# Layer two of a fused kernel: from four blocks of 384 tokens to three of 512, with three pieces of block zero one position later

## The reference, cut to what matters

```
recurrence:  y = mLSTM(q, k, v, input gate, forget gate, output gate)      # per head, over 768 steps
layer one:   x1 = (sigmoid(y @ wg) * (y @ wv)) @ wo                        # 320 -> 1536 -> 320
layer two:   xn = x1 / sqrt(mean(x1 * x1) + 1e-6) * g
             out = (a * sigmoid(a) * (xn @ wv2)) @ wo2    with a = xn @ wg2
```

## Time and profile before

| | |
|---|---|
| median of three runs | 476.69 us (476.38 to 476.94) |
| the profiled execution's own time | 475.81 us |
| its span, first to last instruction | 474.1 us |
| granted TensorE clock, mean | 0.996 |
| layer one's first hidden matmul | 22.66 us |
| layer two's first matmul | 280.88 us |
| layer two's last matmul begins | 471.02 us |

### The profile page before, as it was taken

How to read it: one execution, slowest core, us unless ns; L and a number is a source line. 1 busy time by engine, 2 the same in 40 slices (tenths; PEclk the granted TensorE clock), 3 DMA queues, 4 the chain that set the end, 5 groups by cost and what they waited for, 6 DMA issues and landing times.

```text
span 474.1 us, 9969 instructions
## 1 busy us (share of the span) xinstructions
PE 467.4 (99%) x4115; PEld 455.1 (96%) x4115; DVE 236.0 (50%) x515; ACT 201.0 (42%) x407; POOL 104.1 (22%) x144
## 2 busy tenths in 40 slices
PE   8999999999999999999999999999999999999997
PEld 3899989999999999999999999999999999999997
DVE  8848865562866175435534525650455045504550
ACT  7878446623462636154416743430243024302430
POOL 5979910211101110100014967000000000000000
PEclk9899999999999999999999999999999999999999
DMA  7674720211122012101141520000000100010001
GB/s 245 211 244 145 177 64 29 63 44 43 44 74 61 1 45 58 46 1 35 67 151 52 182 85 1 2 15 29 1 1 7 37 1 3 4 39 2 1 4 39
DMA packets 11475, 27.92 MB, mean 59 GB/s; under 512 B 1526, under 2 KB 5830, under 8 KB 11430
## 3 DMA queue, kind: packets, MB, share of 16 engines
q1 hardware_dynamic: 11110, 27.20, 18.3%
q10 hardware_dynamic: 320, 0.08, 0.1%
HBM read 25.23 MB, written 1.97 MB: 57 GB/s over the span
## 4 chain that ended last, share of the span: by engine, by line
PE 89%; POOL 5%; DVE 3%; ACT 1%; DMA 1%; issue 1%; POOLq 0%; ACTq 0%
PE bank L1055 27%; PE bank L1006 10%; PE bank L1007 9%; PE bank L1075 9%; PE bank L1077 8%; PE bank L1076 8%; PE bank L1009 6%; PE bank L954 3%; PE bank L927 2%; POOL wgv_lo L415 2%; PE bank L1085 2%; PE bank L874 2%; PE bank L946 1%; POOL wgv_hi L418 1%; DMA raw_x<-in_w_o 1%; PE bank L905 1%
## 5 line engine op out<-in xcount | busy, mean ns | idle before, releaser
L1006 PE MATMUL bank<-x_hi,wgv_hi 128*128 128x256 f32 x432 | 121.1, 290 | 0.3 <-DVE x_lo L786 0.3
L1007 PE MATMUL bank<-x_lo,wgv_hi 128*128 128x256 f32 x432 | 118.0, 283 | 0.0
L609 ACT ACTIVATE sg<-bank 128x256 f32<-128x256 f32 (+1 forms) x120 | 51.1, 426 | 151.8 <-PE bank L1007 74.9
L1075 PE MATMUL bank<-wo_hi,h_hi 128*128 128x320 f32 x288 | 90.1, 313 | 0.0
L829 DVE TENSOR_TENSOR hf<-sg,bank 128x256 f32<-128x256 f32 (+1 forms) x120 | 56.7, 473 | 65.1 <-ACT sg L609 62.1
L1055 PE MATMUL bank<-x_hi,wgv_hi 64*128 64x384 f32 x576 | 89.0, 333 | 0.0
L1077 PE MATMUL bank<-wo_hi,h_lo 128*128 128x320 f32 x288 | 89.0, 309 | 0.0
L1076 PE MATMUL bank<-wo_lo,h_hi 128*128 128x320 f32 x288 | 89.0, 309 | 0.0
L1006 PEld LDWEIGHTS bank<-x_hi,wgv_hi 128*128 128x128 f32 x432 | 82.7, 191 | 1.5 <-DVE x_lo L786 0.4
L1007 PEld LDWEIGHTS bank<-x_lo,wgv_hi 128*128 128x128 f32 x432 | 82.7, 191 | 0.0
L1009 PE MATMUL bank<-x_hi,wgv_lo 128*128 128x256 f32 x288 | 81.5, 283 | 0.0
(11 more groups left out here) (125 smaller groups left out, 516.9 us busy)
## 6 DMA issues: line engine op xcount, KB each, us to landing
step<-in_w_gv SPq DMA_DIRECT2D x7, 576.0 KB, 3.8
step<-in_vok SPq DMA_DIRECT2D x12, 324.0 KB, 3.6
step<-in_qk_t SPq DMA_DIRECT2D x24, 160.0 KB
raw_x<-in_w_gv SPq DMA_DIRECT2D x5, 576.0 KB, 4.9
raw_p<-in_w_gv SPq DMA_DIRECT2D x4, 576.0 KB, 4.8
y<-y_tok SPq DMA_DIRECT2D x12, 160.0 KB, 1.8
step<-in_vok SPq DMA_DIRECT2D x10, 180.0 KB, 4.5
step<-in_q_t SPq DMA_DIRECT2D x10, 180.0 KB, 2.5
```

Source lines behind the costliest of these rows:

```text
L609: act.activation(sg[:, f % 2, 0:w], g_view(lay, n), ACT.Sigmoid).then_inc(sg_done, 1)
L1006: pe.matmul(ps, wgv_hi[:, wc, s, cs], x_hi[:, xs, s, :], start=(s == 0), stop=False)
L1007: mm = pe.matmul(ps, wgv_hi[:, wc, s, cs], x_lo[:, xs, s, :], start=False, stop=(s == 2))
L1075: pe.matmul(ps, h[0][:, f, ts], wo_hi[:, f, :], start=(f == 0), stop=False)
```

## The change

Layer two takes four tiles, 512 tokens, per block, in three blocks. The inner values of 512 tokens need more room: f = 0 to 8 stay in `h_hi` and `h_lo`, f = 9 to 11 go to `d_rhs` (high) and to the place of the second `step` buffer (low), and `hf` of layer two goes to the place of `d_lhs`. The fourth projected tile goes out through `num`. As the second `step` buffer is written early in layer two, the weight chunks use the buffers in another order (`RAW1`): chunks 8 and 11 use `raw_p`, so chunk 11 is loaded when chunk 8 is split (before: when chunk 6 was). The last two O pieces stand behind the first and second projected tile of block zero, in banks 0 and 1, and a second or third block waits for both at its start. In block zero of layer one, T of tile 3 moves from slot 12 to slot 13 (on DVE between sub-steps 2 and 3 of A), F of position 2 from slot 13 to 14 and R from slot 14 to 15. The diff, cut:

```diff
-T1 = 3
+T1 = 4
 N1 = T1 * P
 NB1 = NT // T1
+HF = 9
...
 FIRST = [[], [("S", 2)], [], [("K", 2), ("N", 2)], [("Y", 2)], [("D", 3)], [], [("S", 3), ("T", 2)], [],
-         [("K", 3), ("N", 3)], [("Y", 3)], [], [("T", 3), ("A", 2, 0), ("A", 2, 1)],
-         [("A", 2, 2), ("A", 2, 3), ("A", 2, 4), ("F", 2)], [("R", 2)], []]
+         [("K", 3), ("N", 3)], [("Y", 3)], [], [("A", 2, 0), ("A", 2, 1)],
+         [("A", 2, 2), ("T", 3), ("A", 2, 3), ("A", 2, 4)], [("F", 2)], [("R", 2)]]
...
-        h_hi = sb("h_hi", [P, NF * N1], F32R)
-        h_lo = sb("h_lo", [P, NF * N1], F32R)
+        h_hi = sb("h_hi", [P, HF * N1], F32R)
+        h_lo = sb("h_lo", [P, HF * N1], F32R)
...
-        hf = sb("hf", [P, 2, N1], F32)
-        y_tok = sb("y_tok", [P, T1, 3 * P], F32)
+        hf = sb("hf", [P, 2 * N0], F32)
+        y_tok = sb("y_tok", [P, 1 + B, 3 * P], F32)
...
+            over("pad_step", [P, QK + QT + VOK], F32)
+            more_lo = over("more_lo", [P, QK + QT + VOK], F32R)
+            over("pad_rhs", [P, R, P], F32R)
+            hf1 = over("hf1", [P, 2 * N1], F32)
         step = [sb(f"step{b}", [P, QK + QT + VOK], F32) for b in range(B)]
         d_rhs = sb("d_rhs", [P, R, P], F32R)
...
+        more = [d_rhs[:, :, :].rearrange("p r t -> p (r t)"), more_lo]
+        RAW1 = [0, 1, 2, 3, 4, 0, 1, 2, 4, 0, 1, 4]
+
+        def h_view(lay, low, f):
+            t = (h_hi, h_lo)[low]
+            if lay == 0:
+                return t[:, f * N0:(f + 1) * N0]
+            return t[:, f * N1:(f + 1) * N1] if f < HF else more[low][:, (f - HF) * N1:(f - HF + 1) * N1]
...
+        def y_out(t):
+            return y_tok[:, t, 0:DM] if t <= B else num[:, 0:DM]
...
+        def o_bank(n):
+
+            return bank[7] if n < NT - B else bank[n - (NT - B)]
...
             def load_raw1(c):
-                s = c % len(raw1)
-                if c >= len(raw1):
-                    sp.wait_ge(split1, c - len(raw1) + 1)
+                s = RAW1[c]
+                if s in RAW1[0:c]:
+                    sp.wait_ge(split1, c - RAW1[0:c][::-1].index(s))
...
                 for t in range(T1):
-                    if k == 0 and t < B:
-                        piece(("O", NT - B + t))
                     act.wait_ge(o_done, NT + T1 * k + t + 1)
...
-                    act.activation(y_tok[:, t, 0:DM], o_view(1, T1 * k + t), ACT.Copy).then_inc(oe_done, 1)
+                    act.activation(y_out(t), o_view(1, T1 * k + t), ACT.Copy).then_inc(oe_done, 1)
+                    if k == 0 and t < B:
+                        piece(("O", NT - B + t))
...
-                    if n == NT - B:
-
-                        pe.wait_ge(hf_done, F1 + NF - 2)
-                    turn(bank[7], 1 + n % B).then_inc(ot_done, 1)
+                    if n >= NT - B:
+
+                        pe.wait_ge(hf_done, F1 + NF - 1)
+                    turn(o_bank(n), 1 + n % B).then_inc(ot_done, 1)
...
-                            pe.wait_ge(x2_done, max(T1 * (k + 1), NT - B))
+                            pe.wait_ge(x2_done, NT if k else NT - B)
...
                         else:
-                            pe.wait_ge(x2_done, NT)
                             pe.wait_ge(oe_done, T1 * k)
...
                 for t in range(T1):
-                    if k == 0 and t < B:
-
-                        piece(("O", NT - B + t))
                     for half in range(2):
                         project(1, k, t, half)
+                    if k == 0 and t < B:
+                        piece(("O", NT - B + t))
```

More of the change, by code:

```diff
@@ L112, in mlstm_moe_kernel @@
                 first.append(under(f"first{b}", [P, NF * N0], F32R))
-                tails.append(under(f"tail{b}", [P, NF * (N1 - N0)]))
+                tails.append(under(f"tail{b}", [P, HF * N1 - NF * N0]))
         x_hi = sb("x_hi", [P, NT, 3, P], F32R)
         x_lo = sb("x_lo", [P, NT, 3, P], F32R)
-        h_hi = sb("h_hi", [P, NF * N1], F32R)
-        h_lo = sb("h_lo", [P, NF * N1], F32R)
+        h_hi = sb("h_hi", [P, HF * N1], F32R)
+        h_lo = sb("h_lo", [P, HF * N1], F32R)
         wgv_hi = sb("wgv_hi", [P, GVC, 3, CW], F32R)
@@ L122, in mlstm_moe_kernel @@
         raw_p = sb("raw_p", [P, 3 * CW], F32)
-        sg = sb("sg", [P, 2, N1], F32)
-        hf = sb("hf", [P, 2, N1], F32)
-        y_tok = sb("y_tok", [P, T1, 3 * P], F32)
+        sg = sb("sg", [P, 2 * N1], F32)
+        hf = sb("hf", [P, 2 * N0], F32)
+        y_tok = sb("y_tok", [P, 1 + B, 3 * P], F32)
         g_row = sb("g_row", [P, DM], F32)
@@ L130, in mlstm_moe_kernel, with over @@
         QK, QT, VOK = 2 * NG * P + 2 * P, NG * P, HE + DM + KN
+        with ExitStack() as late:
+            def over(name, shape, dt):
+                return late.enter_context(nc.sbuf_tensor(name, shape, dt))
+            over("pad_step", [P, QK + QT + VOK], F32)
+            more_lo = over("more_lo", [P, QK + QT + VOK], F32R)
+            over("pad_rhs", [P, R, P], F32R)
+            hf1 = over("hf1", [P, 2 * N1], F32)
         step = [sb(f"step{b}", [P, QK + QT + VOK], F32) for b in range(B)]
@@ L167, in mlstm_moe_kernel, with sg_view, hf_view @@
         raw1 = [step[s // 2][:, s % 2 * 3 * CW:(s % 2 + 1) * 3 * CW] for s in range(4)] + [raw_p[:, :]]
-        h0 = [t[:, 0:NF * N0].rearrange("p (f t) -> p f t", t=N0) for t in (h_hi, h_lo)]
-        h1 = [t[:, :].rearrange("p (f t) -> p f t", t=N1) for t in (h_hi, h_lo)]
+        more = [d_rhs[:, :, :].rearrange("p r t -> p (r t)"), more_lo]
[5 more added lines that the diff above has]
+            return t[:, f * N1:(f + 1) * N1] if f < HF else more[low][:, (f - HF) * N1:(f - HF + 1) * N1]
+        def sg_view(lay, f):
+            w = (N0, N1)[lay]
+            return sg[:, f % 2 * w:(f % 2 + 1) * w]
+        def hf_view(lay, f):
+            w = (N0, N1)[lay]
+            return (hf, hf1)[lay][:, f % 2 * w:(f % 2 + 1) * w]
+        def y_out(t):
+            return y_tok[:, t, 0:DM] if t <= B else num[:, 0:DM]
         bank = [ctx.enter_context(nc.psum_tensor(f"bank{i}", [P, 512], F32)) for i in range(8)]
@@ L190, in raw_of @@
         def raw_of(lay, c):
-            ring = (raw0, raw1)[lay]
-            r = ring[c % len(ring)]
+            r = raw0[c % len(raw0)] if lay == 0 else raw1[RAW1[c]]
             if c < GVC:
@@ L376, in _ @@
                     row = m % B * S + m // B * P
-                    sp.dma_start(out[row:row + P, :], y_tok[:, t, 0:DM]).then_inc(out_sent[t], 16)
+                    sp.dma_start(out[row:row + P, :], y_out(t)).then_inc(out_sent[t], 16)
             for t in range(T1):
@@ L513, in high @@
             def high(lay, c):
-                ring, whi = ((raw0_in, whi0), (raw1_in, whi1))[lay]
-                s = c % len(ring)
-                act.wait_ge(ring[s], 16 * (c // len(ring) + 1))
+                whi = (whi0, whi1)[lay]
+                if lay == 0:
+                    act.wait_ge(raw0_in[c % len(raw0)], 16 * (c // len(raw0) + 1))
+                else:
+                    act.wait_ge(raw1_in[RAW1[c]], 16 * RAW1[0:c + 1].count(RAW1[c]))
                 if c < GVC:
@@ L571, in piece @@
                     act.wait_ge(ot_done, n + 1)
-                    act.activation(x_hi[:, n, :, :], t_view(bank[7]), ACT.Copy).then_inc(xh2_done, 1)
+                    act.activation(x_hi[:, n, :, :], t_view(o_bank(n)), ACT.Copy).then_inc(xh2_done, 1)
             act.wait_ge(consts, 1)
@@ L604, in sigmoid @@
             def sigmoid(lay, n, f):
-                w = (N0, N1)[lay]
                 act.wait_ge(g_done if lay else v_done, n + 1)
@@ L608, in sigmoid @@
                     act.wait_ge(hf_done, n - 1)
-                act.activation(sg[:, f % 2, 0:w], g_view(lay, n), ACT.Sigmoid).then_inc(sg_done, 1)
+                act.activation(sg_view(lay, f), g_view(lay, n), ACT.Sigmoid).then_inc(sg_done, 1)
             def h_high(lay, n, f):
-                w, h = ((N0, h0), (N1, h1))[lay]
                 act.wait_ge(hf_done, n + 1)
@@ L618, in h_high @@
                         act.wait_ge(o_done, before)
-                act.activation(h[0][:, f, :], hf[:, f % 2, 0:w], ACT.Copy).then_inc(hhi_done, 1)
+                act.activation(h_view(lay, 0, f), hf_view(lay, f), ACT.Copy).then_inc(hhi_done, 1)
             for k in range(NB0):
@@ L650, in _ @@
                 for t in range(T1):
-                    if k == 0 and t < B:
-                        piece(("O", NT - B + t))
                     act.wait_ge(o_done, NT + T1 * k + t + 1)
-                    if k == 0 and t:
+                    if k == 0 and 0 < t <= B:
                         act.wait_ge(ot_done, NT - B + t)
@@ L789, in piece @@
                     dve.wait_ge(xh2_done, n + 1)
-                    dve.tensor_tensor(x_lo[:, n, :, :], t_view(bank[7]), x_hi[:, n, :, :].bitcast(F32),
+                    dve.tensor_tensor(x_lo[:, n, :, :], t_view(o_bank(n)), x_hi[:, n, :, :].bitcast(F32),
                                       ALU.subtract).then_inc(x2_done, 1)
@@ L819, in gate @@
             def gate(lay, n, f):
```

(20 more changed lines are left out.)

## The result

| | median, us | runs |
|---|---|---|
| before | 476.79 | 476.38 to 476.94 (4) |
| after | 472.63 | 472.42 to 474.14 (4) |
| ratio | 0.9921 | 95% interval 0.9899 to 0.9942 |

The kernel is 4.2 us faster; 4.9 were forecast (471.8), and the time lies in the range. The interval of the ratio allows 2.8 to 4.8.

The account below looks back on a forecast made before the run. PE, busy for 99% of the span, was taken to bound the kernel. Gains of 2.9 + 2.0 = 4.9 us took 475.81 to 470.9, or 471.8 us with the median's 0.9 carried over; range 470.5 to 474.3.

Parts of the forecast that it names:

- The step of 512 columns: Layer two's pairs: a step takes 213.3 + 14.5 = 227.8 ns, the excess belonging to the instruction.
- Rival (a): Layer two's pairs: the excess grows with the columns, 232.7 ns a step, time 474.5 us; chance 0.10.
- (c): Layer two's pairs: halves writing two whole banks cost more, slower than before from 238.6 ns a step; chance 0.04.
- part one: Layer two at 512 columns: 540 steps instead of 720, gain 2.9 us, 2.7 of it in the steps.
- Layer two: All of layer two: three blocks plus the two O pieces take 187.6 us, against 190.47 before.
- ACT and DVE beside it: Longer tiles in layer two: multiply 689 ns at 512, hidden; at least 0.4 us spare at a block's end.
- Chunk 11: Early layer two: first sigmoid 8.5 us in, first hf at 10.5, wanted at 13.7; 3 us spare, no cost.
- Part two: End of block zero: moving T, F and R removes PE's waits, gain 2.0 us, bounds 0 and 2.0.
- the forecast's 11.5 us: Block zero's first projection to block one: work, T, R and refills without waiting, 11.5 of 13.57 us.
- two close places: Block zero's end: f = 11's low part even with its demand; sums ready at 65.6, R reached about 66.2.
- What is late next: F to D's exponentials, block one: done by 73.15, S reached at 73.4, 0.2 to 0.3 us spare.
- Rival (b): Block one: F's landing or the exponentials stop PE at D or S for 2 us, time 473.8; chance 0.10.

Follow-up runs that it names:

- e8: Changed kernel with fifteen matmuls on zeros filling the start, behind the scores, the first T, N and K; 471.68 us against 477.05, ratio 0.9898.
- E6: Changed kernel with chunk 11 in chunk 10's buffer instead of chunk 8's, so its load waits for two more splits; 478.11 us.
- e4: Kernel before with T alone moved to slot 13, F and R where they were; 477.40 us against 477.05, ratio 1.0012.
- e5: Kernel before with F and R alone moved to slots 14 and 15, T at slot 12; 476.09 us, ratio 0.9992.
- e3: Kernel before with the new slots of block zero, layer two unchanged; 475.05 us against 477.04, ratio 0.9952.
- e1: Changed kernel again, no edit, on another chip; 472.47 us against 477.04 for the kernel before, ratio 0.9902.
- e2: Changed kernel with the old slots of block zero (T 12, F 13, R 14); 474.36 us against 477.04 before, ratio 0.9954.
- e10: Changed kernel with seven matmuls on zeros in the start's waits, beside the kernel before with the same filling; 471.44 us, ratio 0.9888.

## Why the prediction was right, point by point

- **The step of 512 columns**: 227.8 ns forecast; 41.00 / 180 = 227.8 measured. Rival (a), 232.7, and (c), over 238, are out. Not all of the 14.5 ns belongs to the instruction, though: inside a block 28 steps take 6.35 us in after (starts from 427.62 to 433.97), 226.8 ns each, and 13 take 2.25 in before (357.83 to 360.08), 173.1. That leaves 13.1 to 13.5 ns beyond the columns, as at 256 and 320; the other 0.2 us of a block's pairs lie at its edges. The forecast held because a block has 180 steps and its edges before and after. Full weight loads are not what makes the excess: PEld was busy for 99% of the first block's pairs before and for 85% after, and the excess is the same. (Of part one's gain the steps are 180 x 14.5 ns = 2.6 us, not the 2.7 of the prediction.) The first and last starts of the two counts, before, then after:

```profile
357.83 0.33 PE L1055 MATMUL bank<-x_lo,wgv_hi 64*128 64x384 f32 x2
...
360.08 0.34 PE L1055 MATMUL bank<-x_hi,wgv_lo 64*128 64x384 f32 x2
```

```profile
427.62 0.39 PE L1082 MATMUL bank<-x_hi,wgv_hi 64*128 64x512 f32 x2
...
433.97 0.39 PE L1082 MATMUL bank<-x_lo,wgv_hi 64*128 64x512 f32 x2
```

  The Trainium skill ("TensorE: Matmul & The Clock Gate", "Back-to-back issue gap") gives an isolated warm matmul about 2.5 ns beyond its columns; by that I estimate 215.8 ns a step and 38.8 us for a block's pairs. These float32 streams disagree, with 41.00. The bfloat16 matmuls of 512 columns that fill the start agree: four in e8 take 1.03 us, the last of them 0.38, so they follow one another in 217 ns, 4 beyond their columns. Why the two kinds differ no run shows:

```profile
20.40 1.03 PE L1117 MATMUL bank<-inter 128*128 128x512 bf16 x4
```

- **Layer two**: 187.6 forecast, 187.74 measured; gain 2.7 instead of 2.9. The 0.13 lies in the transitions: the O pieces take 0.64 instead of 0.59, the first and the last block a few hundredths more.
- **ACT and DVE beside it**: the multiply at 512 was put at 689 ns and takes 687. At a block's end, the low parts of f = 10 and 11, then the first of PE's matmuls for f = 11:

```profile
388.66 1.47 DVE L862 TENSOR_TENSOR more_lo<-hf,d_rhs 128x512 fp32r<-128x512 f32 x2
```

```profile
390.72 0.31 PE L1101 MATMUL bank<-wo_hi,d_rhs 128*128 128x320 f32 x1
```

They are ready at 390.13, and f = 11 is wanted at 390.72: 0.6 spare, 0.4 at least forecast.
- **Chunk 11**: first sigmoid 8.5 us into layer two forecast, 289.92 - 281.77 = 8.15 measured, and the first `hf` at 291.94, 10.2 in, with 3.5 spare:

```profile
289.01 1.01 ACT L558 ACTIVATE wo_hi<-raw_p 128x960 fp32r<-128x960 f32 x1 [3.93 <-DMA raw_p<-in_w_o]
289.92 1.06 ACT L641 ACTIVATE sg<-bank 128x512 f32<-128x512 f32 x2
```

```profile
291.25 0.69 DVE L858 TENSOR_TENSOR hf<-sg,bank 128x512 f32<-128x512 f32 x1
```

E6 shows what the spare is for: a landing of 5.2 us, as there, would still be covered.
- **Part two**: 2.0 forecast, 1.98 measured between the two points and 1.88 with the refill behind R, which the forecast's 11.5 us contain and after's 11.59 do not; e4 and e5 show that it takes both moves. Of the two close places one lost a little. f = 11's low part was to be even with its demand, a tenth of a microsecond late at most; it ended at 62.87, 4.83 after the first projection, and T began 5.43 after it instead of 5.28, so PE lost 0.15. In e3 T begins 5.28 after it, and nothing is lost. The sums came at 68.44 and R began at 69.17, unwaited:

```profile
62.45 0.42 DVE L862 TENSOR_TENSOR h_lo<-hf,h_hi 128x256 fp32r<-128x256 f32 x1
...
68.26 0.18 DVE L750 TENSOR_TENSOR l_end<-l_r,sel 16x32 f32<-16x32 f32 x1
```

- **What is late next**: F, table load and D's exponentials:

```profile
68.26 1.17 ACTq L584 DMA_DIRECT2D d_rhs<-l_row  x2
...
69.46 1.28 ACT L590 ACT_TABLE_LOAD   x1 [4.56 <-issue]
...
74.47 1.09 ACT L568 ACTIVATE tail<-bank 128x512 f32<-128x512 f32 x2
```

From load to exponentials it took 5.01 us, 5.48 before; the exponentials ended at 75.56 and S began at 76.36. Spare 0.8, since the waits for PE that I left in the chain were gone. Rival (b) is out.
- **What the forecast had too large**, though the range held: 4.9 us, where the traces of before and e1 say 4.6 from the first hidden matmul on. Part one is 0.1 to 0.2 smaller, by the transitions above; part two is 0.15 smaller, by the wait for f = 11. About 0.1 more lies outside the span: time less span has medians of 1.84 to 1.86 us in after, e1, e2 and e6 and 1.74 to 1.77 in before, e3, e4 and e5. So it comes with part one, and why stays open. From 4.6 to the 4.2 of the first comparison it is a matter of a few runs: its interval reaches 4.8, and the changed kernel's four were at clocks of 0.993 and 0.989, while those of before's four are not known. The sum also carries over the 0.9 us by which before's profiled execution lies below the median. That had no reason behind it: 475.8 is what before takes at 0.996, the highest clock it showed, and its median is a mixture (0.986 to 0.996 in e1). It did little harm, since both kernels showed such mixtures, and e1's medians are 4.6 apart like the traces.

## What to carry to other kernels

Read the spacing of a matmul stream at several widths: if what is left beyond the columns is the same, it is a price per instruction of that stream, and wider tiles save it for every instruction that goes, 14.5 ns times 180 here with a block's edges in it, as long as the other engines' longer tiles still fit at a block's end. Two waits that hang on one chain have to be moved together; either alone can be worth nothing. And before a few tenths of a per cent are compared, look at the granted clock of each execution: here two executions of the changed kernel, alike from the first hidden matmul on, differ by 1.6 us in the start alone, and the runs of either kernel spread over 2 us and more.

## What the runs showed of the hardware that I had not expected

- PE ran at the lower of its two clocks (1.2 GHz) while the rows call it busy for 4.00 of 4.00 us (after, 18 to 22 us). Ahead of it lay a wait of 0.76 us and then 32 matmuls of only 41 columns, during which it fell (the line below). With seven wide matmuls in the waits the mean granted clock was 1.0 in four of e10's six runs.

```profile
13.88 6.35 PE L982 MATMUL bank<-step,tail 128*128 128x41 f32 x32 [0.76 <-DVE tail L762]
```

- A stop of 3.45 us in dense work (e6) was followed, 1.3 us after work had begun again, by 3.4 us at 1.2 GHz.
- One transfer of 480 KB, chunk 11's, took 3.1 us to land in the changed kernel and 5.2 in e6, where it goes to another buffer, with no other load issued beside it in either (one execution each).
